# A fused attention and expert kernel on one core: order of the first loads, routing in pairs of blocks, three tiles of the first expert taken ahead of the tables

## The reference

```python
k_sum = k.reshape(B, H, nb, block, D).max(axis=3)
v_sum = v.reshape(B, H, nb, block, D).mean(axis=3)
...
a = a / (np.sum(a, axis=-1, keepdims=True) + 1e-09)
v_all = np.concatenate([v, v_sum], axis=2)
x = np.matmul(a, v_all)                      # then (B*S, H*D)
logits = x @ w_gate + modality_bias[modality_id]
e_idx = np.argmax(logits, axis=1)
for e in range(E):
    mask = e_idx == e
    h = np.maximum(x[mask] @ w1[e], 0.0)
    out[mask] = gate_w[mask, None] * (h @ w2[e])
h = np.maximum(out @ w_in, 0.0)
return (h * h @ w_out)
```

## Time and profile before

| | us |
|---|---|
| three runs, median (lowest to highest) | 591.02 (585.96 to 595.11) |
| the profiled execution | 588.5 |
| its span, first to last instruction | 586.8 |
| PE busy / DVE / ACT / POOL | 531.4 / 230.8 / 183.5 / 90.1 |
| mean granted clock of PE | 0.946 |

### The profile page before, as it was taken

One profiled execution on the slowest core, in us unless ns is written; L12 is line 12 of the kernel. 1 busy time (PEld: TensorE's weight loads), 2 busy tenths in 40 slices (PEclk: granted clock), 3 DMA queues, 4 the chain that ended last, 5 costly groups with the idle time before them and its releaser, 6 DMA issues.

```text
span 586.8 us, 9477 instructions
## 1 busy us (share of the span) xinstructions
PE 531.4 (91%) x3092; PEld 424.9 (72%) x3094; DVE 230.8 (39%) x450; ACT 183.5 (31%) x345; POOL 90.1 (15%) x104
## 2 busy tenths in 40 slices
PE   7769999689999969998369999999999999999996
PEld 3558787467888758877247888877888887888884
DVE  4766777836121252622552223223223224221222
ACT  2446653226221261622512222222221224122221
POOL 3545263104100031040360000002000000000000
PEclk9689995979999979999859999999999999999999
DMA  8994783591811108134130000004000001000001
GB/s 299 334 281 136 224 272 130 172 349 37 315 57 40 36 18 328 47 141 199 54 89 20 1 0 1 0 2 143 0 0 0 0 0 71 0 0 0 0 0 71
DMA packets 19273, 56.71 MB, mean 97 GB/s; under 512 B 2352, under 2 KB 2608, under 8 KB 18480
## 3 DMA queue, kind: packets, MB, share of 16 engines
q1 hardware_dynamic: 12048, 29.83, 15.8%
q0 software_dynamic: 4608, 23.07, 10.7%
q10 hardware_dynamic: 2592, 3.48, 1.6%
HBM read 42.48 MB, written 13.89 MB: 96 GB/s over the span
## 4 chain that ended last, share of the span: by engine, by line
PE 75%; DVE 7%; DMA 6%; ACT 4%; issue 3%; POOL 1%; ACTq 1%; SPq 1%; DVEq 0%; POOLq 0%
PE psum L1436 8%; PE psum L1438 8%; PE psum L1437 8%; PE psum L1417 7%; PE psum L1418 7%; PE psum L1419 7%; PE psum L1336 4%; PE psum L1337 3%; PE psum L1338 3%; PE psum L1350 3%; PE psum L1351 3%; PE psum L1352 3%; DMA q_in<-in_q 3%; ACT W L522 2%; DMA X<-in_vT 2%
## 5 line engine op out<-in xcount | busy, mean ns | idle before, releaser
L1151 DVE TENSOR_TENSOR sq<-r_sb 128x512 f32<-128x512 f32 x48 | 33.2, 692 | 155.7 <-ACT r_sb L630 155.7
L630 ACT ACTIVATE r_sb<-psum 128x512 f32<-128x512 f32 x48 | 28.8, 599 | 162.1 <-PE psum L1419 162.1
L1417 PE MATMUL psum<-z_hi,W 128*128 128x512 f32 x192 | 77.0, 401 | 0.8 <-DVE z_lo L1135 0.8
L1418 PE MATMUL psum<-z_lo,W 128*128 128x512 f32 x192 | 76.8, 400 | 0.0
L1436 PE MATMUL psum<-W,s_hi 128*128 128x512 f32 x192 | 75.9, 395 | 1.1 <-DVE s_lo L1153 1.1
L1419 PE MATMUL psum<-z_hi,W 128*128 128x512 f32 x192 | 76.8, 400 | 0.0
L1438 PE MATMUL psum<-W,s_lo 128*128 128x512 f32 x192 | 75.7, 394 | 0.0
L1437 PE MATMUL psum<-W,s_hi 128*128 128x512 f32 x192 | 75.3, 392 | 0.0
L1336 PE MATMUL psum<-W,x_hi 128*128 (+1 forms) x104 | 45.0, 433 | 11.7 <-DVE W L913 5.9
L1350 PE MATMUL psum<-W,h_hi 128*128 (+1 forms) x104 | 42.1, 405 | 4.8 <-DVE h_lo L921 4.7
L1153 DVE TENSOR_TENSOR s_lo<-sq,s_hi 128x512 fp32r<-128x512 f32 x48 | 33.2, 693 | 33.5 <-ACT s_hi L632 33.5
(11 more groups left out here) (194 smaller groups left out, 724.9 us busy)
## 6 DMA issues: line engine op xcount, KB each, us to landing
raw<-in_w POOLq DMA_DIRECT2D x4, 2048.0 KB, 12.6
raw<-in_w_io POOLq DMA_DIRECT2D x4, 2048.0 KB, 9.9
v_in<-in_v SPq DMA_DIRECT2D x12, 390.0 KB, 7.2
raw<-in_w SPq DMA_DIRECT2D x8, 512.0 KB, 9.6
x_in<-xs_d SPq DMA_DIRECT2D x14, 256.0 KB, 2.8
kT<-in_kT SPq DMA_DIRECT2D x8, 400.0 KB, 8.1
q_in<-in_q SPq DMA_DIRECT2D x12, 256.0 KB, 6.9
X<-in_vT SPq DMA_DIRECT2D x2, 1536.0 KB, 9.8
```

What stands on the lines that cost most here:

```text
L1417: pe.matmul(bank[f % 2][:, :], wh, z_hi[:, k, :], start=(k == 0), stop=False)
L1418: pe.matmul(bank[f % 2][:, :], wh, z_lo[:, k, :], start=False, stop=False)
```

## The change

- Loads: `q_in` runs one block further ahead; the keys of batch 1 come ahead of its value sums' source `vT`; `vT` of batch 1 comes behind `v_in` of block 3. The zero fill of `xs_d` goes from iteration 4 to 6. POOL's `sum_values` and PE's `value_sums(1)` come two `keys_of` and one iteration later.
- Routing groups are (0,2), (2,2), (4,2), (6,2), (8,2), (10,2). Ranks of three groups are now made inside the loop (scores 7, 9, 11) in place of two (scores 7, 11). `choose` comes one iteration earlier, `settle` in DVE's iteration 8, after group 1 in place of group 2. Scatters 0 and 1 stand inside POOL's loop.
- The chosen expert's first weights are asked for in iteration 8 in place of 9; three of the four low parts of w1 are made without DVE (`EARLY` 3).
- `SPEC` = 3: tiles 0, 1 and 2 are taken to be the chosen expert's. SP loads tiles 0 and 1 in iteration 10, tile 2 after the last scatter. `layer1(0)` begins behind `x_turn(10)`, and what was left of the tail (gate logits of blocks 9, 10, 11, `x_turn(11)`, ranks of group 4) stands between its four steps; ranks of group 5 follow `h_transpose(0)`. The `keep_warm` products are gone. Layer 1 of tiles 0, 1, 2 and layer 2 of 0 and 1 run before PE waits for `tab`. The second expert's weights are split at tile 2.
- DVE computes the table after `h_low(0)` and the low parts, `slots` and `tables` after `moe_step(1)`. `TILES` is 21 in place of 20.

```diff
-RGROUPS = ((0, 2), (2, 4), (6, 2), (8, 2), (10, 2))
-SETTLED = 3
-EARLY = 2
+SPEC = 3
+RGROUPS = ((0, 2), (2, 2), (4, 2), (6, 2), (8, 2), (10, 2))
+SETTLED = 2
+INLOOP = 3
+EARLY = 3
@@ SP
             load_q(0)
+            load_q(1)
             load_values(0)
-            load_q(1)
+            load_q(2)
             load_v(0)
-            load_q(2)
+            load_q(3)
             load_v(1)
-            load_v(2)
-            load_q(3)
-            load_values(1)
             for c in range(PAIRS):
                 load_keys(1, c)
+            load_q(4)
+            load_v(2)
+            load_q(5)
             load_v(3)
-            load_q(4)
-            load_q(5)
+            load_values(1)
...
+                if i == NB - 2:
+                    sp.wait_ge(sem["zfill"], 16)
+                    sp.wait_ge(sem["scat_a"], sum(RGROUPS[SETTLED - 1]) * 16)
+                    sp.wait_ge(sem["x0"], 1)
+                    for t in range(2):
+                        row = ...
+                        sp.dma_start(x_in[t][:, :], xs_d[bass.ds(row, P), :]).then_inc(s_xs[t], 16)
@@ POOL
-            for i in range(RING, NBS):
+            for i in range(RING, NBS + 2):
                 keys_of(i)
             sum_values()
-            for i in range(NBS, NBS + RING):
-                keys_of(i)
+            keys_of(NBS + 2)
             sums_of(NBS)
             sums_of(NBS + 1)
+            scatter(0)
             keys_of(NBS + RING)
             sums_of(NBS + 2)
             keys_of(NB - 2)
-            scatter(0)
             sums_of(NBS + 3)
+            scatter(1)
             keys_of(NB - 1)
...
             low_0(0)
             low_0(1)
-            for g in range(1, len(RGROUPS)):
+            scatter(2)
+            low_0(2)
+            for g in range(3, len(RGROUPS)):
                 scatter(g)
@@ DVE, settle
-                r(dve.tensor_scalar(seen_n[:, 1:2], seen_n[:, 0:1], float(P), float(P), ALU.is_ge, ALU.mult))
-                dve.tensor_tensor(table[:, T_X0:T_X0 + 1], ...).then_inc(sem["x0"], 1)
-                r(dve.tensor_scalar(seen_n[:, 0:1], ...))
-                r(dve.tensor_scalar(skip[:, :], ...))
+                for n in range(2):
+                    r(dve.tensor_scalar(seen_t[:, n:n + 1], seen_n[:, 0:1], float(P * (n + 1)), None, ALU.is_lt))
+                r(dve.tensor_reduce(seen_n[:, 1:2], seen_t[:, :], AX.X, ALU.add))
+                r(dve.tensor_scalar(skip[:, :], ...))
+                r(dve.tensor_scalar(spec_c[:, 0:1], ...))
+                r(dve.tensor_scalar(spec_r[:, :], ...))
+                r(dve.tensor_scalar(spec_r[:, :], ...))
+                dve.tensor_copy(table[:, T_X0:T_X0 + 2], spec_r[:, 0:2]).then_inc(sem["x0"], 1)
+                r(dve.tensor_scalar(least[:, :], ...))
@@ DVE, behind the loop, as it is after
+            rank_copy(3); route_b(3)
+            logits(NB - 4); x_low(0); norm(NB - 1); low_a(0, 0, (EARLY,))
+            logits(NB - 3); route_a(4)
+            logits(NB - 2); rank_copy(4); route_b(4)
+            logits(NB - 1); route_a(5); x_low(1)
+            rank_copy(5); route_b(5); settle_last()
+            low_a(0, 0, (PARTS,)); low_a(0, 0, (PARTS + 1,))
+            h_low(0)
+            low_a(0, 0, (PARTS + 2,)); low_a(0, 0, (PARTS + 3,))
...
+            moe_step(1, 0, 0)
...
+            tables()
...
+            moe_step(2, 1, 0)
+            low_a(1, 1)
@@ PE
+            ranks(3)
             pe.wait_ge(sem["pt0"], NB)
             x_transpose(0, 0, 1)
-            keep_warm(3)
-            ranks(4)
+            values(NB - 1)
+            x_turn(NB - 2)
+            pe.wait_ge(sem["rk"], 4)
...
-            layer1(0, 0, 1)
-            pe.wait_ge(sem["rk"], len(RGROUPS))
+            layer1(0, 0, 1, between=((1, tail_a), (2, tail_b), (3, tail_c), (KD, tail_d)))
+            x_transpose(1, 1, 1)
+            pe.wait_ge(sem["rk"], 5)
             h_transpose(0)
+            ranks(5)
+            layer1(1, 0, 1)
             layer2(0, 0, 1)
-            x_transpose(1, 1, 1)
+            x_transpose(2, 0, 2)
+            h_transpose(1)
+            layer1(2, 0, 1)
+            x_transpose(3, 1, 2)
+            layer2(1, 0, 1)
+            h_transpose(2)
             pe.wait_ge(sem["tab"], 1)
```

More of the change, by code:

```diff
@@ L296, in build @@
         ksum kw sc mx ex tr0 tr1 pt0 pt1 pv norm xt xtc lg rank route vtsum vtsum_p sums vm vsum
-        y_row rows slots rout oh tab n_run e0 x0 warm early lsub scat_b scat_c zfill_y
+        y_row rows slots rout oh tab n_run e0 x0 warm early lsub scat_b scat_c scat_d scat_e x2 zfill_y
         raw0 raw1 zfill scat_a x_t x_h x_l l1 relu ht hh hl l2 y sh sla slbv slbp yall
@@ L552, in _ @@
             high_0(5)
-            x_high(0)
-            for part in range(6, 2 * PARTS):
-                high_0(part)
+            high_0(6)
             def split_w(slot, k):
@@ L833, in row_max @@
                     logits(i - 5)
-                for g in range(SETTLED - 1):
+                for g in range(INLOOP):
                     if i == routed_at(g) + 2:
@@ L998, in _ @@
             route_b(3)
-            dve.wait_ge(sem["lg"], NB)
-            logits(NB - 1)
+            dve.wait_ge(sem["lg"], NB - 3)
+            logits(NB - 4)
+            x_low(0)
+            norm(NB - 1)
+            low_a(0, 0, (EARLY,))
+            dve.wait_ge(sem["lg"], NB - 2)
+            logits(NB - 3)
             route_a(4)
-            low_a(0, 0, (EARLY + 1,))
-            x_low(0)
+            dve.wait_ge(sem["lg"], NB - 1)
+            logits(NB - 2)
             dve.wait_ge(sem["rank"], 5)
@@ L1006, in _ @@
             route_b(4)
+            dve.wait_ge(sem["lg"], NB)
+            logits(NB - 1)
+            route_a(5)
+            x_low(1)
+            dve.wait_ge(sem["rank"], 6)
+            rank_copy(5)
+            route_b(5)
+            settle_last()
             low_a(0, 0, (PARTS,))
+            low_a(0, 0, (PARTS + 1,))
+            h_low(0)
+            low_a(0, 0, (PARTS + 2,))
+            low_a(0, 0, (PARTS + 3,))
             T1 = TILES + 1
@@ L1046, in _ @@
             dve.tensor_copy(table[:, T_ROW:T_ROW + T1], row_t[:, 1, :]).then_inc(sem["rows"], 1)
-            h_low(0)
-            low_a(0, 0, (PARTS + 1, PARTS + 2))
-            r(dve.tensor_tensor(used_e[:, :], used[:, :], cfv("run"), ALU.mult))
-            r(dve.tensor_tensor(exp_w[:, 0, :, :], wide(first[:, 1, :], 1, E), wide(cfv("run"), 2, E), ALU.is_equal))
-            r(dve.tensor_tensor(exp_w[:, 1, :, :], exp_w[:, 0, :, :], wide(used_e[:, :], 1, E), ALU.mult))
-            r(dve.tensor_reduce(exp_f[:, :], exp_w[:, 1, :, :], AX.X, ALU.add))
-            dve.tensor_copy(table[:, T_EXP:T_EXP + E], exp_f[:, :]).then_inc(sem["slots"], 1)
             def y_copy(t, dst):
@@ L1093, in tables @@
                 dve.wait_ge(sem["tab"], 1)
-            moe_step(0)
+            moe_step(1, 0, 0)
+            r(dve.tensor_tensor(used_e[:, :], used[:, :], cfv("run"), ALU.mult))
+            r(dve.tensor_tensor(exp_w[:, 0, :, :], wide(first[:, 1, :], 1, E), wide(cfv("run"), 2, E), ALU.is_equal))
+            r(dve.tensor_tensor(exp_w[:, 1, :, :], exp_w[:, 0, :, :], wide(used_e[:, :], 1, E), ALU.mult))
+            r(dve.tensor_reduce(exp_f[:, :], exp_w[:, 1, :, :], AX.X, ALU.add))
+            dve.tensor_copy(table[:, T_EXP:T_EXP + E], exp_f[:, :]).then_inc(sem["slots"], 1)
+            tables()
             n_t = n_tiles(dve)
@@ L1294, in x_transpose @@
                 ins.then_inc(sem["x_t"], 1)
-            def keep_warm(n):
-                for _ in range(n):
-                    pe.matmul(bank[4][:, :], warm[:, 0:P], warm[:, :], start=True, stop=True)
             x_turn(NB - 3)
@@ L1340, in layer1 @@
                             ins.then_inc(sem["l1"], 1)
+                for at, do in between:
+                    if at == KD:
+                        do()
             def layer2(t, slot, run):
```

218 lines of the change are left out of this document (111 added, 107 removed).

## The result

| | before | after |
|---|---|---|
| median, 20 runs each | 588.82 us (584.83 to 595.11) | 594.53 us (590.47 to 596.28) |
| ratio of the runs | | 1.009, interval 1.0067 to 1.0113 |
| profiled execution: span | 586.8 us | 590.0 us |
| mean granted clock | 0.946 | 0.947 |

The forecast was 578, with 569 to 588 as its range. The measured time lies outside of it and on the other side. A ratio compares executions made side by side and leaves out those more than 1.5% above the fastest of their kernel, so it is not the quotient of the two medians.

What follows compares the result with a forecast made beforehand. Loads bound the kernel from 20 to 40 us, waits before tile 3, PE from there on. The terms -6.1 + 3.1 + 1.0 - 8.0 - 3.1 = -13.1 gave 575.4 on the profiled 588.5, 578 on the median; range 569 to 588.

Steps and rivals of the forecast that it cites:

- part 1: Loads ahead of block 4: with `vT` and values moved behind, the wait for `q_in` goes; -6.1 us, bounds -2 and -7.5.
- part 2: Routing inside the loop: added PE waits and DVE lag, +3.1 us (bounds +1 and +6), plus +1.0 for held operations.
- part 3: Tile 0: `layer1(0)` starts 11.1 us earlier but runs longer, 10.2 us; -8.0 us, bounds -10.5 and -4.
- part 4: Tiles 1 to 3: from the end of `layer1(0)`, 34.8 us in place of 37.9; -3.1 us, bounds -6.5 and +2.
- I add +1.0, two operations of route and settle held up by half a us each; bounds 0 and +3: In the loop: DVE's small operations delayed beside POOL's copies, priced from two `bias_v` at 0.72 us each; +1.0 us.
- PE waits for POOL's keys in blocks 8 to 9 for over 2 us: In the loop: one of the signs that would show the forecast wrong.
- DVE bounds the new tail: Rival: ranks, route steps and table in one DVE queue, each small operation waiting longer; +7 us, 585; chance 0.12.
- The signs of the forecast (70.5, 83.5, 93.5): Expected times in us in the profile after: scores 11, first product of tile 0, and its last product.
- The new wait for `x_low(2)`: Ahead of `layer1(2)`: PE waits 3.7 us for DVE, then 10 products at the lower clock, +2.0 us.
- L: The end of `layer1(0)`, from which times in tiles 1 to 3 were counted; `layer1(3)` was to start at L+34.0.
- Nothing of the change reaches there, nor the dense layer: From tile 3 on: PE is the chain, so whatever is won before is kept to the end one for one.
- Slower than before: Rival: PE clock stays at its lower level from the tail to tile 3, 24 us against 4.2 counted; 598; chance 0.05.

Runs made afterwards that it cites:

- e3: After with POOL's keys of block 11 ahead of scatter 1 and its first low part held until DVE's first maximum of `row_max(10)`: 589.59 us, 1.0004 to before.
- e2: After with the old order of loads: 593.93 us, ratio 1.0071 to before.
- e1: Before with the new order of loads alone, including its later value sums and zero fill: 588.41 us, ratio 1.0009 to before.
- e6: Before with its table eight words longer, buffers 32 bytes later as in after: 591.61 us, ratio 1.0045 to before.
- e7: After with five laps of the tile loop in place of nine, so no empty laps ahead of the last layer 2: 590.59 us, 1.0048 to before.
- e5: After with its table five words longer, buffers 64 bytes later than in before: 583.38 us, ratio 0.9937 to before.
- e9: Before with its table 16 words longer, buffers 64 bytes later: 586.49 us, ratio 0.9901 to before.
- e10: After with its table 24 words longer, buffers 128 bytes later than in before: 592.51 us, ratio 1.0035 to before.
- e8: e3 with each of POOL's three low parts in four pieces of 256 columns: 588.09 us, ratio 1.0004 to before.
- e13: After at the address of e5, POOL's instructions reordered, low parts in pieces (as in e3 and e8, with further moves), and five laps: 581.54 us, 0.9811 to before.
- e4: After with the five expert-table operations moved earlier, so the second expert's weights are asked for sooner: 593.82 us, 1.0114 to before.

## Why the prediction was wrong

In the profiled executions the steps stand so (us; negative is a gain):

| step | forecast | measured |
|---|---|---|
| to scores 6 (part 1) | -6.1 | -4.0 |
| scores 6 to scores 11 (part 2) | +4.1 | +12.0 |
| scores 11 to the last product of tile 0 (part 3) | -8.0 | -5.1 |
| from there to `x_transpose(5)` (part 4) | -3.1 | -3.2 |
| from there to the end | 0 | +3.5 |
| sum | -13.1 | +3.2 |

The steps that failed are part 2 (7.9 of the 16.3 us between forecast and profile), "from there to the end" (3.5), part 3 (2.9) and part 1 (2.1).

**Part 2 was mis-sized**, 12.0 for 4.1, and beyond its upper bound of 6. The 12.0 are 7.2 us of idle time and 4.9 of longer PE time. Three terms failed.

The first is "I add +1.0, two operations of route and settle held up by half a us each; bounds 0 and +3". In the changed kernel the held operations took 11.3 us longer than the same shapes undisturbed (some 0.17 each), against 2.9 in the kernel before: 5.7 of it between scores 6 and 11, where before has 0.5, and 2.1 at 90.83; the rest lies ahead of 26 us, as most of before's does. The wait ahead of scores 11 is 4.83 us and was 1.00; 3.7 of the 3.8 us more are lines 971 and 972.

The rule that spoke against the change was cited there, and the row that it was priced by was misread. "0.72 us each (1.44 for two)" is a mean: the first of the two `bias_v` took 0.26 us, as without POOL, and the second 1.15. The next two operations of before, the second one on 8 columns, were held as long:

```profile
22.05 0.99 DVE L870 TENSOR_TENSOR bias_t<-bias_v 128x96 f32<-128x96 f32 x1
23.07 0.90 DVE L872 COPY end_row<-cr 128x8 f32<-128x8 f32 x1
```

So the price of a whole instruction of POOL stood in the trace before. The Trainium skill ("SBUF — State Buffer", section "SBUF: two separate sides") says that where a VectorE operation with two SBUF inputs meets a GpSimd one that reads SBUF, the loser waits for the whole instruction. The trace agrees (line 903 has two such inputs and ends 0.04 us behind the low part beside it), and has one more case: at 73.13 DVE, with one tensor and a scalar from SBUF, waited through three of POOL's instructions in a row, two of the keys and the low part. And POOL's longest, the low part of 2.34 us, was not on my list of those beside which `settle` could fall. e3 takes this one hold away, for some 0.9%; smaller ones stay in it.

The second is that the forecast gave the added waits of the loop no clock. It priced the lower clock for tiles 0 to 2, and none behind waits of 1 us in the loop. But the values at 51.07 take 2.00 us behind a wait of 1.27, and scores 9 and 11 take 1.88 in place of 1.05. In the stretch from scores 6 to 11 this is the 4.9 us of longer PE time, as much as the holds.

The third is a term put at nothing: `choose` comes one iteration earlier, into the one that has `route_b(0)`. The thirteen small operations of the two stand there in a row, from 54.94 to 59.05, two of them held by 1.5 us together, and PE waits 1.46 us at 61.08. In before they stood in two iterations and PE did not wait. In e2, where neither of the two is held, the wait is 0.38. What the forecast did count came true: the wait of the new group is 1.09 us (forecast 1.2), and without the hold `settle` costs 1.3 us ahead of scores 11 (e3: 1.41 + 0.85 - 1.00; forecast 1.5).

The loop is the steadiest part of the result. From scores 6 to 11 four of the six profiles with before's loop and loads have 27.04 or 27.05 us (the others 28.93 and 31.73), the six with after's loop 37.7 to 41.0, and the five with after's loop without the hold 36.0 to 37.9. The sign "PE waits for POOL's keys in blocks 8 to 9 for over 2 us" looked for a late POOL; what came was a DVE held by POOL, two blocks later. The rival "DVE bounds the new tail" had the right engine and the wrong place: it is the loop.

**Part 1** had the right mechanism and the wrong worth. The idle goes, as said; but -6.1 measured -4.0 here, and in eleven other profiles with the new loads scores 4 stand anywhere from 31.81 to 35.06, because in six of them scores 3 at 29 us already run at the lower clock. Scores 6 stand at 42.6 to 45.3 us with the new loads and at 44.3 to 47.0 with the old, with medians 2.8 us apart. In the median nothing is left of it (e1, e2). The sum also took for granted that a gain at scores 6 is passed on whole through the tail. It isn't: in e1 the 1.1 us won at scores 11 were lost at the next meeting of DVE and POOL.

**Part 3** went by its own distances: from scores 11 the first product of tile 0 was to come at 83.5 - 70.5 = 13.0 us, and came 16.0 behind; its length was to be 10.2 and was 9.7. In that stretch the rows show the hold of 2.25 at 90.83 and a clock of 0.82. Of the 14.2 us by which the start came later than its sign, 11.2 stood already at scores 11 and 3.0 arose here. The signs of the forecast (70.5, 83.5, 93.5) also stand 1 us ahead of its own sum: they leave out the +1.0 for held operations.

**Part 4** is right in this profile by two errors that cancel, one of them luck. The new wait for `x_low(2)` was to be 3.7 us and is 3.16, at 19.4 us behind L (forecast 19.2). The clock did not fall behind it, and the 2.0 us that I took for it were not due, so that `layer1(3)` began at L+32.0 (139.39) in place of L+34.0. But in nine of the eleven profiles with this wait (3.16 to 3.41 us) it did fall, and tile 2 then took 1.4 us longer and more. Against this the second expert's weights came late, 15.67 us from a request at 132.04, and took back 2.5 us (the round from `x_transpose(4)` at 145.07 to `x_transpose(5)` at 160.09 is 15.0 us). The forecast named that load as a bound and did not count it. Where the clock falls most of this lateness goes, so the two do not add up. That the length of an idle does not settle what the clock does stood in the trace before: "an idle 2 us (106 to 108)" is the middle of one of 2.69, behind which it stayed full, and behind 2.87 it fell.

```profile
108.52 0.50 PE L1350 MATMUL psum<-W,h_hi 128*128 128x512 f32 x1 [2.69 <-DVE h_lo L921]
```

**"Nothing of the change reaches there, nor the dense layer"** is the step that was wrong without any bound, and it had nothing behind it but a stretch. It cost twice: 32 bytes of address (0.45% by e6, half of the result) and one more skipped step ahead of the last layer 2 (2.2 us, e7). "From tile 3 on PE is busy without a gap" holds for the 160 to 200 us of the earlier trace rows alone. Behind them, at tile 8, while the weights of a further expert are split, PE of the kernel before stands idle for 5.88 us, put down to DVE's low parts, and the clock is down for 6.8 us:

```profile
210.26 0.79 PE L1336 MATMUL psum<-W,x_hi 128*128 x1 [5.88 <-DVE W L913]
```

This round takes 21.25 us in before, 20.13 in after, and 19.9 to 21.4 over all profiles, of both kernels alike: 1.1 us was won there by chance, and without it the +3.5 were 4.6. At equal addresses the change costs some 0.4%: e5 against e9, 0.9937 to 0.9901, and after against e6, 1.009 to 1.0045. Each of the two is about as large as its uncertainty, and the pairs come from different batches on different chips: e10 has after's round within 0.01 us and a dense group only 0.3 shorter, and its ratio is 1.0035, not 1.009.

Of the rivals none is what happened. "Slower than before" named the clock from the tail to tile 3; the clock fell in the loop and the tail, four times between 50 and 101 us, and from 101 us to 108 it was 0.98; behind the wait for `x_low(2)` it stayed up in this profile, but not in most others. What stays open: how much of the cost of the loop a single hold carries once the clock that falls behind it is counted, since each sets off the next; why the gains of e8 and e13 in their profiles do not show in the medians; and 2.5 of the 5.7 us between the medians, which the two profiles do not show.

## What to carry to other kernels

Before small operations go into a loop, list every instruction of the other engine that is seen to hold such operations up (here GpSimd's), the longest ones and those back to back first, and price a meeting at their whole length; read this price from single operations, since a row of two hides that one was held and one was not. Where the order can't exclude a meeting, cut the long instruction into pieces. Give a term to every operation that changes its iteration, not to the new ones alone. An edit that lengthens any table moves all buffers behind it: compare the rate of an untouched loop before and after (here 12.34 and 12.51) before the rest is explained, and try two or three paddings. Before "nothing reaches there" is written of three quarters of a kernel, read all of its stretches. A gain of a few us in one profile, ahead of a part where the clock and waits of other engines decide, is no gain until the median shows it.

## What the runs showed of the hardware that I had not expected

- TensorE's rate on fp32r products at full granted clock depends on where the buffers in SBUF start (those behind the table; the weights did not move): 12.25 to 12.52 us a tile, 90.86 to 93.28 us a dense group, the same again 256 bytes later. It was worth 1.0% in the kernel before (e9).
- A VectorE operation on 3 columns stood for 3.35 us while three instructions of GpSimd ran one behind the other, and others of that size for 2.25 and 2.28 beside a low part (after at 90.83, e1 at 79.44). Of e8's pieces a reduction of the same size took no harm: line 909 took 0.17 us between two held operations, at 90.69, while POOL's pieces ran.
- The granted clock fell behind an idle of 2.75 us (279.00) and stayed full behind one of 3.16 (126.85). The same wait of 3.17 us was followed by a fall in e4 (128.07) and in e10 (127.76): the same instructions behind the same idle can come out either way.
